# q and the result turned by VectorE in 32x32 blocks that the DMAs put into place, with q's low part on GpSimd

## What is computed

```python
# attention; q: 12288 x 128, keys: 96 x 8 = 768
kv_pool = kv.reshape(B, H//4, 4, W//4, 4, C).mean(axis=(2, 4))
k = v = kv_pool.reshape(B, -1, C) @ w_sr
s = (q @ k.T) / sqrt(C);  a = exp(s - s.max(-1));  a /= a.sum(-1) + 1e-9
x = a @ v                                            # 12288 x 128
# MLP 1 (d_ff 2048), then MLP 2 (d_ff 2048)
h = x @ w_in1;  y = (h * clip(h + 3, 0, 6) / 6) @ w_out1
h = y @ w_in2;  g = where(h >= 1, h, where(h <= -1, 0, (h + 1)**2 / 4))
out = g @ w_out2
```

## Time and profile before

| what | us |
|---|---|
| time, median of 3 runs | 1386.23 (1386.03 to 1388.38) |
| profiled execution: span from first to last instruction | 1385.0 |
| TensorE busy | 1366.2 (99%) |
| VectorE busy | 1166.3 (84%) |
| ScalarE busy | 1153.9 (83%) |
| GpSimd busy | 205.6 (15%) |

### The profile page before, as it was taken

How to read it: one execution, slowest core, us unless ns; L and a number is a source line. 1 busy time by engine, 2 the same in 40 slices (tenths; PEclk the granted TensorE clock), 3 DMA queues, 4 the chain that set the end, 5 groups by cost and what they waited for, 6 DMA issues and landing times.

```text
span 1385.0 us, 19432 instructions
## 1 busy us (share of the span) xinstructions
PE 1366.2 (99%) x6517; PEld 1144.3 (83%) x6517; DVE 1166.3 (84%) x1286; ACT 1153.9 (83%) x1429; POOL 205.6 (15%) x152
## 2 busy tenths in 40 slices
PE   7999999999999999999999999999999999999998
PEld 6888888887888888888888888888888888888886
DVE  6777777777988888888888888888888888888888
ACT  1677777667889899899989989898998999899896
POOL 0566655451000000000000000000000000000012
PEclk9999999999999999999999999999999999999999
DMA  9000000000000000000000000000000000000000
GB/s 328 24 23 23 23 23 23 23 1 1 0 1 8 8 8 1 8 8 8 0 8 8 8 8 0 8 8 8 8 0 8 8 8 1 7 8 8 9 0 23
DMA packets 10154, 23.48 MB, mean 17 GB/s; under 512 B 1040, under 2 KB 1168, under 8 KB 9872
## 3 DMA queue, kind: packets, MB, share of 16 engines
q1 hardware_dynamic: 10128, 23.14, 4.8%
HBM read 16.84 MB, written 6.29 MB: 17 GB/s over the span
## 4 chain that ended last, share of the span: by engine, by line
PE 94%; DVE 4%; ACT 1%; issue 0%; DMA 0%; ACTq 0%; DVEq 0%
PE ps L704 37%; PE ps L770 36%; PE ps L640 8%; PE ps L616 7%; PE ps L627 4%; DVE probs L492 1%; DVE g_lo L552 1%; PE ps L602 1%; PE ps L791 1%; DVE gate L546 1%; ACT g_hi L424 0%; DMA x_all<-in_kv 0%; ACT pt_hi L336 0%; DVE pt_lo L484 0%; DVE negmax L470 0%
## 5 line engine op out<-in xcount | busy, mean ns | idle before, releaser
L552 DVE TENSOR_TENSOR g_lo<-gate,g_hi 128x1024 fp32r<-128x1024 f32 x384 | 479.5, 1249 | 108.6 <-ACT g_hi L424 108.5
L546 DVE SCALAR_TENSOR_TENSOR gate<-gate,ps 128x1024 f32<-128x1024 f32 x384 | 451.6, 1214 | 2.9 <-ACT gate L407 2.7
L424 ACT ACTIVATE g_hi<-gate 128x1024 fp32r<-128x1024 f32 x384 | 405.9, 1057 | 1.2 <-DVE gate L546 1.2
L770 PE MATMUL ps<-g_hi,w_hi 128*128 128x512 f32 x768 | 299.2, 390 | 0.6 <-DVE g_lo L552 0.6
L770 PE MATMUL ps<-g_lo,w_hi 128*128 128x512 f32 x768 | 299.0, 389 | 0.0
L770 PE MATMUL ps<-g_hi,w_lo 128*128 128x512 f32 x768 | 298.8, 389 | 0.0
L409 ACT ACTIVATE gate<-ps 128x1024 f32<-128x1024 f32 x192 | 197.7, 1030 | 83.0 <-PE ps L704 79.0
L407 ACT ACTIVATE gate<-ps 128x1024 f32<-128x1024 f32 x192 | 195.9, 1020 | 11.5 <-PE ps L704 10.9
L418 ACT ACTIVATE gate<-gate 128x1024 f32<-128x1024 f32 x185 | 195.2, 1055 | 0.0
L283 POOL TENSOR_TENSOR x_lo<-x_all,x_hi 128x512 fp32r<-128x512 f32 x24 | 31.2, 1300 | 936.3 <-ACT x_hi L388 936.3
L770 PEld LDWEIGHTS ps<-g_hi,w_hi 128*128 128x128 f32 x768 | 144.2, 188 | 31.2 <-DVE g_lo L552 1.0
(11 more groups left out here) (64 smaller groups left out, 1620.7 us busy)
## 6 DMA issues: line engine op xcount, KB each, us to landing
x_all<-in_kv SPq DMA_DIRECT2D x12, 512.0 KB, 8.9
q_in<-in_q SPq DMA_DIRECT2D x24, 256.0 KB, 2.6
out<-out_sb SPq DMA_DIRECT2D x24, 256.0 KB, 2.0
w_raw<-in_moe_w_in SPq DMA_DIRECT2D x2, 1024.0 KB, 17.3
probs<-in_w_sr SPq DMA_DIRECT2D x1, 64.0 KB, 12.8
w_raw<-in_moe_w_out SPq DMA_DIRECT2D x2, 0.5 KB, 13.5
```

The lines of the kernel that those rows point to most:

```text
L424: nc.scalar.activation(g_hi[:, n % RING, :], gate[:, n % RING, :], ACT.Copy).then_inc(g_hi_done, 1)
L546: nc.vector.scalar_tensor_tensor(out=gate[:, n % RING, :], in0=gate[:, n % RING, :], scalar=6.0 if mlp == 1 else 1.0, in1=hidden, op0=ALU. ...
L552: nc.vector.tensor_tensor(g_lo[:, n % RING, :], gate[:, n % RING, :], g_hi[:, n % RING, :].bitcast(F32), ALU.subtract).then_inc(g_lo_done, 1)
L770: last = nc.tensor.matmul(ps[:, y_bank(mlp, t), :], left[:, cols], right[:, n % RING, toks], start=(p == 0 and e == 0 and a == 0), stop=(p ...
```

## The change

1. q is loaded by four DMAs a tile. DMA b fetches the channels 32b to 32b+31 of all 512 tokens into partitions 32b to 32b+31, as 16 groups of 32x32: its runs in memory are 32 values, 128 bytes. The result is stored in the same way by four DMAs a tile.
2. q is turned by one VectorE instruction (`nc.vector.transpose`, 128x512, every 32x32 block by itself) into a new tile `qt` in SBUF, in step c = 1 of its program, between the row maximum and `add_eps`. The four turns on TensorE are gone; at the start five keep-warm turns take the place of four turns and one keep-warm turn. ScalarE makes the high part from `qt`.
3. q's low part moves from VectorE to GpSimd, behind the normalisation of part 2 and ahead of that of part 3.
4. The result is turned by VectorE straight out of the PSUM bank of MLP 2 into `out_sb` in step n. ScalarE's copy to `y_out`, TensorE's turns and the wait for the borrowed bank are gone. The next tile's first output product waits for `out_ready`, which VectorE gives.

```diff
-            sp.dma_start(q_in[:, 0, :], q_tiles[0]).then_inc(q_loaded[0], 16)
-            sp.dma_start(q_in[:, 1, :], q_tiles[1]).then_inc(q_loaded[1], 16)
+            for j in (0, 1):
+                for b in range(QUADS):
+                    sp.dma_start(block_rows(q_in[:, j, :], b), q_blocks[j, b]).then_inc(q_loaded[j], 16)
...
+            def q_low(i, k):
+                pool.wait_ge(qt_hi_done, i + 1 + 2 * k)
+                nc.gpsimd.tensor_tensor(qt_lo[:], qt[:], qt_hi[:].bitcast(F32),
+                                        ALU.subtract).then_inc(qt_lo_done, 1)
...
                     normalise(i, r, k)
                     if splits_weights and r == 1:
                         weights_low(i - 1, k)
+                    if i + 1 < TILES and r == 2:
+                        q_low(i + 1, k)
...
-                nc.scalar.activation(qt_hi[:], ps[:, BANK_Q, :], ACT.Copy).then_inc(qt_hi_done, 1)
+                nc.scalar.activation(qt_hi[:], qt[:], ACT.Copy).then_inc(qt_hi_done, 1)
...
-            def q_low(i, k):
-                dve.wait_ge(qt_hi_done, i + 1 + 2 * k)
-                nc.vector.tensor_tensor(qt_lo[:], ps[:, BANK_Q, :], qt_hi[:].bitcast(F32),
-                                        ALU.subtract).then_inc(qt_lo_done, 1)
+            def turn_q(i, k):
+                dve.wait_ge(q_loaded[i % 2], 16 * QUADS * (i // 2 + 1) + 16 * QUADS * k)
+                if i:
+                    dve.wait_ge(qt_lo_done, i + 2 * k)
+                nc.vector.transpose(qt[:], q_in[:, i % 2, :]).then_inc(qt_done, 1)
...
-                    if after and c == SUB - 1:
-                        q_low(i + 1, k)
+                    if after and c == 1:
+                        turn_q(i + 1, k)
...
-                t = turn_at[n]
-                dve.wait_ge(turned, t + 1 + 2 * k)
+                mlp, t = y_at[n]
+                dve.wait_ge(y_added, slot_of[(2, t, PAIRS - 1)] + 1 + BODY * k)
                 if t >= 2:
-                    dve.wait_ge(stored[t % 2], 16 * (t // 2) + 16 * k)
-                nc.vector.tensor_copy(out_sb[:, t % 2, :], ps[:, turn_bank(n), :]).then_inc(out_ready, 1)
+                    dve.wait_ge(stored[t % 2], 16 * QUADS * (t // 2) + 16 * QUADS * k)
+                nc.vector.transpose(out_sb[:, t % 2, :], ps[:, BANK_Y[2], :]).then_inc(out_ready, 1)
...
-            turn_q(0, 0)
-            keep_warm(1)
+            keep_warm(5)
...
-                    if after and c == SUB - 1:
-                        turn_q(i + 1, k)
...
-                    pe.wait_ge(y_lo_done if mlp == 1 else y_out_done, t + 2 * k)
+                    pe.wait_ge(y_lo_done if mlp == 1 else out_ready, t + 2 * k)
...
-                    for r in range(SUB):
-                        last = nc.tensor.transpose(ps[:, turn_bank(n), r * P:(r + 1) * P],
-                                                   y_out[:, r * P:(r + 1) * P], ident[:])
-                    last.then_inc(turned, 1)
```

More of the change, by code:

```diff
@@ L30 @@
 POOL = 4
+BLK = 32
+GROUPS = TOK // BLK
+QUADS = P // BLK
 def build_program(nc, q, kv, w_sr, w_in1, w_out1, w_in2, w_out2, out):
@@ L93, in pool_squares @@
         return SLOTS - 1 > n >= SLOTS - ALONE and slots[n][2] % 2 == 1
-    STEPS = SLOTS + T_AFTER + 1
+    STEPS = SLOTS + LAG + 1
     BODY = 2 * TILE_SLOTS
@@ L130, in build_program @@
         q_in = sb("q_in", [P, 2, TOK], F32, phase_a)
+        qt = sb("qt", [P, TOK], F32, phase_a)
         qt_hi = sb("qt_hi", [P, TOK], F32R, phase_a)
@@ L182, in build_program, with block_rows @@
         y_hi_done, y_lo_done = sem("y_hi_done"), sem("y_lo_done")
-        y_out_done, turned, out_ready = sem("y_out_done"), sem("turned"), sem("out_ready")
+        out_ready = sem("out_ready")
         stored = [sem("stored0"), sem("stored1")]
-        q_tiles = q.rearrange("o (t p r) c -> t p (o r c)", p=P, r=SUB)
-        out_tiles = out.rearrange("(t p r) c -> t p (r c)", p=P, r=SUB)
+        q_blocks = q.rearrange("o (t g i) (b j) -> t b i (o g) j", i=BLK, j=BLK, g=GROUPS)
+        out_blocks = out.rearrange("(t g i) (b j) -> t b i g j", i=BLK, j=BLK, g=GROUPS)
         kv_rows = kv.rearrange("o (j p) w c -> j p (o w c)", p=P)
         KVW = WW * C
+        def block_rows(tile, b):
+            return tile[b * BLK:(b + 1) * BLK, :].rearrange("i (g j) -> i g j", j=BLK)
         A_LOOPS = (TILES - 2) // 2
@@ L248, in _ @@
                     sp.wait_ge(qt_done, 2 * k + (j - 1))
-                    sp.dma_start(q_in[:, j % 2, :], q_tiles[bass.ds(2 * k + j, 1)].rearrange("o p f -> (o p) f")
-                                 ).then_inc(q_loaded[j % 2], 16)
+                    for b in range(QUADS):
+                        sp.dma_start(block_rows(q_in[:, j % 2, :], b),
+                                     q_blocks[bass.ds(2 * k + j, 1), b].rearrange("o i g j -> (o i) g j")
+                                     ).then_inc(q_loaded[j % 2], 16)
             with sp.Fori(0, TILES // 2) as k:
@@ L254, in _ @@
                     sp.wait_ge(out_ready, 2 * k + (j + 1))
[L255 to L258, removed]
+                    for b in range(QUADS):
+                        sp.dma_start(out_blocks[bass.ds(2 * k + j, 1), b].rearrange("o i g j -> (o i) g j"),
+                                     block_rows(out_sb[:, j, :], b)).then_inc(stored[j], 16)
+            sp.wait_ge(stored[0], 16 * QUADS * (TILES // 2))
+            sp.wait_ge(stored[1], 16 * QUADS * (TILES // 2))
         @block.gpsimd
@@ L428, in step @@
                     gate_input(n, k)
-                if n in y_at:
+                if n in y_at and y_at[n][0] == 1:
                     mlp, t = y_at[n]
@@ L432, in step @@
                     act.wait_ge(y_added, last + 1 + BODY * k)
[L433 to L440, removed]
+                    nc.scalar.activation(y_hi[:, t % 2, :], ps[:, y_bank(1, t), :], ACT.Copy,
+                                         scale=1.0 / 6.0).then_inc(y_hi_done, 1)
                 if n in split_at:
@@ L574, in step @@
                     gate_low(n - SPLIT_LAG, k)
-                if n in turn_at and n != SLOTS - 1:
+                if n in y_at and y_at[n][0] == 2:
                     take_results(n, k)
-                if n == SLOTS - 1 + SPLIT_LAG and SLOTS - 1 in turn_at:
-                    take_results(SLOTS - 1, k)
                 if n < SLOTS and slots[n][0] == 2:
@@ L693, in hidden_block @@
                         pe.wait_ge(g_done, m + 1 + BODY * k)
-                    for d in range(1, 8):
-                        if m is not None and n - d in turn_at and turn_bank(n - d) == 2 * group(n) and n - d > m:
-                            pe.wait_ge(out_ready, turn_at[n - d] + 1 + 2 * k)
                     if p == 0:
```

27 lines of the change are left out of this document (3 added, 24 removed).

## The result

| | before | after |
|---|---|---|
| time, median (lowest to highest) | 1386.13 (1385.08 to 1388.38), 4 runs | 1452.0 (1449.2 to 1453.3), 4 runs |
| profiled execution: span | 1385.0 | 1451.2 |

The change makes the kernel slower: ratio 1.0467, 95% interval 1.0452 to 1.0483. Predicted were 1434.7 in a range of 1426 to 1457. So 17.3 us are missing from the forecast.

A forecast was written before the change was run, and what follows sets the result against it. TensorE, 99% busy, was taken to bound the kernel, with GpSimd making it wait. 1385.0 + 51.3 (attention) - 2.5 - 0.8 (result tiles) + 0.5 (DMAs, tail) = 1433.5 span; median 1434.7, range 1426 to 1457.

The forecast's parts named there:

- GpSimd late with q's low part: Attention: low part ready 10.31 us after TensorE's turn of the first probabilities (T); next scores (S) wait 2.5; attention +51.3.
- The clock: TensorE's granted clock in attention: the sum took no fall behind the new waits, so 0 us.
- rival C: Attention: gaps of 2.5 us drop TensorE to the 1.2 GHz level in 22 iterations, +143, 1578 us; chance 0.03.
- Periods close on themselves: Attention: the wait is paid every iteration; period 14.14 for 11.78 in iterations 1 to 16, 13.56 in 17 to 22.
- The removed turns of q bring nothing: Attention: dropping TensorE's q turns gains 0, since each iteration's end is set by the wait for GpSimd.
- VectorE's turn: VectorE: a 128x512 turn costs what a copy does, 0.65 us; 0.09 added to the attention period.
- Rival A: VectorE turns 4-byte values at half the copy's pace, about 1.25 us for 512: 1457 us; chance 0.12.
- The interleaved result tiles: MLP: TensorE's turns save 0.44, waiting for VectorE loses 0.32; net -0.12 a tile, -2.5 over 21 tiles.
- the forecast's lower bound: MLP result tiles: with VectorE's turn quicker by 0.3 the wait is gone and 21 x 0.44 = 9.2 us are won.
- The two tiles alone: MLP, tiles 21 and 22: ScalarE's 0.5 less and no late wait, about -0.8 us for both.
- The tail: DMAs and end: 1.34 us of copies go, 1.3 of store issues and 0.5 for small runs come; +0.5 (0 to +3).
- the forecast's own bound of 1448: Whole kernel: upper end of the forecast's own range, with VectorE's turn at 0.95, +10.9, and a slow last store.

The follow-up runs named there:

- e1: The changed kernel with idle turns of the identity on TensorE ahead of the scores that wait for q's low part: 1435.36 us, ratio 1.0349.
- e3: The kernel before with the result part of the change alone, q loaded, turned and split as before: 1386.66 us, ratio 0.9998.
- e7: The kernel before with VectorE's turn of the result, put ahead of the low part of slot n-2, and q's rows loaded in 512-byte runs: 1376.73 us, ratio 0.9929.
- e8: As e7, with the result's turn of the two tiles that run alone one gate function earlier still: 1374.31 us, ratio 0.9909 to the kernel before.
- e5: The changed kernel with GpSimd's low part of q behind part 1 and the weight piece behind part 3: 1390.4 us, ratio 1.0027.
- e10: The changed kernel with GpSimd's weight piece behind part 3, q's low part left behind part 2: 1431.34 us, ratio 1.0324.
- e2: The changed kernel with q's low part back on VectorE, in step c = 3, out of SBUF: 1391.14 us, ratio 1.0031.
- e11: The kernel before with the q part of the change alone, the result turned by TensorE and stored in 512-byte runs: 1445.65 us, ratio 1.0419.
- e4: The kernel before with each q load and each store cut into four DMAs of 128-byte runs, data landing as before: 1388.81 us, ratio 1.0014.

## Why the prediction came out as it did

- **GpSimd late with q's low part: right, in place and size.** The wait is at L613, 23 times. The undisturbed periods are 14.01 (forecast 14.14) and 13.52 (13.56). S stands at T + 10.42, forecast T + 10.45; the other 0.10 is the restart that I added to the 3.59 from S to T, and which doesn't show there (3.58). I forecast waits of 2.5 and 2.1; they are 2.00 and 1.51, since TensorE now first waits 0.29 for a turned block, which its q turns had covered. That moves time from one wait to another and does not change the period. In iteration 0, S came at 43.87 for 42.14, +1.7 where I had +2.85, because its normalisations all stood some 1 us earlier than I had them (part 0 at 36.42, before at 37.42); but from S to T it took 4.0 for 2.4, at the lower clock: +3.4 in all.
- **The clock: the step that failed.** I gave it as rival C, all or nothing, 143 us at a chance of 0.03, and put 0 into the sum. It came in part: in 10 of 16 iterations about 1.5 us each (one 2.8), 16.4 in the profile; e1, with iteration 0's share, gives 16.6 between the medians. My evidence against it was one wait of 2.28 in iteration 0 that drew no fall. One row can't say this: here 6 waits of 2.00 in 16 drew none either, and in e3, e7 and e8, where TensorE's program in iteration 0 is before's, the same wait of 2.28 to 2.29 did draw one. And the price was wrong: the clock came back within some 3 us of work, in the iteration of 2.8 within some 6, and not at the next iteration. The wait of e3 and a stretch behind it (columns as in the stretches of after above):

```profile
40.78 0.77 PE L609 MATMUL ps<-kt_hi,qt_hi 128*128 128x384 f32 x2 [2.28 <-DVE qt_lo L460]
...
42.00:43.00 1.00, 1.00 (x5) 1.00 (x5) 0.13 (x1) 0.00 (x0) 1.00 (x1) 0.50 0.00 0
```

- **Periods close on themselves: right.** Nothing upstream won time back. e5 and e10 show it from both sides: 11.83 with the low part behind part 1, 13.53 with it behind part 2, each the same from one iteration to the next but for e10's two longer ones.
- **The removed turns of q bring nothing: right, but my reason covered only this order.** In e2, with the wait for GpSimd gone, they still brought nothing. They had been filling a hole of TensorE.
- **VectorE's turn: right.** 701 ns out of SBUF, 709 out of PSUM, for a copy's 684. Rival A is gone. What I gave as speaking for it was misread: 0.95 for 512 values, against the copy's 0.65, is two thirds of the copy's pace and not nearly half.
- **The interleaved result tiles: right.** -0.10 a tile, forecast -0.12. e7 shows that the whole 0.44 is there once VectorE's turn stands a place earlier; the forecast's lower bound had that gain, by a quicker turn.
- **The two tiles alone: missed.** I forecast -0.8 and no late wait. There the first output product comes one step after the sum is complete, not two, but VectorE still put the low part of slot n-2 ahead: the turn starts at 1407.39 and TensorE idles 1.72 and 1.71. From the last T to the end the span grew by 0.5; with -2.1 for 21 tiles and +0.1 for the tail that leaves +2.5 for these two. I had read the step numbers and not laid them beside VectorE's order.
- **The tail: small.** The last output product starts 5.18 ahead of the end, before 5.11: ScalarE's copy and TensorE's turns are gone, -1.3, and the four small-run stores take 1.4 more from VectorE's last instruction to the end. The loads in the loop are hidden.

Sum of the misses: clock in the loop +16.4, undisturbed periods -2.6, iteration 0 +0.5, tiles 21 and 22 +3.3, the 21 tiles +0.4, tail -0.4: 17.6, against 1451.2 - 1433.5 = 17.7. That the time lies in the range is luck: it is above the forecast's own bound of 1448, and only the room given to rival A, which didn't happen, reaches it. The error was the treatment of the clock.

## What to carry to other kernels

Moving work to an engine that is 15% busy is priced by the place in its program, not by its share: the same instruction on GpSimd cost 61 us behind part 2 and the weight piece, and left no wait behind part 1 (e5). When an instruction leaves the bound engine, look for what its slot was hiding, and when a result changes hands, put the new owner's instruction ahead of anything that isn't due: e7 and e8 won 12 us over e3 by doing so. A new wait of about 2 us in every iteration of TensorE is not priced by its length alone; filling it with idle turns gave back 16.6 us.

## What the runs showed of the hardware

- Behind waits of the same length the granted clock did not always fall. Waits of 2.00 us: behind 10 of 16 in after, 8 of 16 in e11. Waits of 1.51 us: behind none of 6 in after, 1 of 6 in e11, 1 of 22 in e10. Waits of 2.28 to 2.29 us in iteration 0: none in before and e4, one each in e3, e7 and e8. Where it fell in the loop of after, the lowered stretch began at about the first matmul behind the wait in five cases and 1.2 to 1.5 us after it in five, and cost about 1.5 us, once 2.8. What decides it in a single iteration stays open. The Trainium skill (TensorE: Matmul & The Clock Gate, What's actually happening) has the lower level as the default, which activity releases; the rows at 0.50 behind idle time agree, and the 6 of 16 waits without a fall show that it takes more than one such row to price it.
- VectorE's subtraction of 128x512 with both operands in SBUF took 0.67 where GpSimd was idle when it began, and 1.23 where it began beside a GpSimd instruction; the next GpSimd instruction took 1.92 for 1.47 (e2).
- 101648 packets of under 512 B, 1040 before, cost nothing where they were hidden (e4): a 64 KB load in 128-byte runs landed in 2.2 us, a 256 KB one in 2.6 before.
